# A Fourier mixing layer and two feed-forward layers on one core: the first element's DMA queue, keep-warm counts and weight-pair slots rearranged

## The reference

```python
def reference(x, filt_r, filt_i, w_in, w_out, alpha, w2_in, w2_out):
    # x: 2 x 3008 x 256, float32
    X = np.fft.rfft(x, axis=1)
    y = np.fft.irfft(X * (filt_r + 1j * filt_i)[None], n=3008, axis=1)
    t = y.reshape(6016, 256)
    h = t @ w_in                                  # 256 x 2048
    t = (np.maximum(h, 0) + alpha * np.minimum(h, 0)) @ w_out
    h = np.maximum(t @ w2_in, 0)
    return (h * h) @ w2_out
```

## Time and profile before

| | us |
|---|---|
| median of 3 runs (lowest to highest) | 1151.18 (1150.83 to 1153.68) |
| the profiled execution, its own time | 1149.17 |
| its span, first to last instruction | 1147.4 |
| TensorE busy | 1122.2 (98% of the span) |
| VectorE busy | 956.7 (83%) |
| ScalarE busy | 655.5 (57%) |
| GpSimd busy | 592.8 (52%) |

### The profile page before, as it was taken

How to read it: one execution, slowest core, us unless ns; L and a number is a source line. 1 busy time by engine, 2 the same in 40 slices (tenths; PEclk the granted TensorE clock), 3 DMA queues, 4 the chain that set the end, 5 groups by cost and what they waited for, 6 DMA issues and landing times.

```text
span 1147.4 us, 17088 instructions
## 1 busy us (share of the span) xinstructions
PE 1122.2 (98%) x6867; PEld 980.2 (85%) x6867; DVE 956.7 (83%) x1110; ACT 655.5 (57%) x769; POOL 592.8 (52%) x434
## 2 busy tenths in 40 slices
PE   7979999999999999999999999999999999999997
PEld 3456888888899999999999899999999999999996
DVE  0659788897989888888988988888888898888987
ACT  4737556565655556555556556555565555555553
POOL 0405544656555565565565654555455455555443
PEclk9999999999999999999999999999999999999999
DMA  9874352453204313312216801101100110110100
GB/s 260 267 232 117 83 137 70 117 127 96 58 29 133 83 51 83 83 51 83 83 51 225 313 7 37 37 1 36 37 16 22 36 36 1 37 37 1 37 19 18
DMA packets 63296, 93.16 MB, mean 81 GB/s; under 512 B 5232, under 2 KB 50288, under 8 KB 63216
## 3 DMA queue, kind: packets, MB, share of 16 engines
q1 hardware_dynamic: 63216, 92.06, 27.5%
HBM read 55.60 MB, written 36.44 MB: 80 GB/s over the span
## 4 chain that ended last, share of the span: by engine, by line
PE 90%; DVE 5%; issue 3%; POOL 1%; DMA 1%; ACT 1%; DVEq 0%; SPq 0%; PEldq 0%; POOLq 0%
PE bank L892 14%; PE bank L897 14%; PE bank L893 14%; PE bank L920 13%; PE bank L918 13%; PE bank L930 13%; PE bank L870 3%; DVE g_lo L739 1%; PE bank L830 1%; PE bank L832 1%; PE bank L844 1%; PE bank L838 1%; DVE g_raw L758 1%; DVE w_lo L685 1%; PE bank L812 1%
## 5 line engine op out<-in xcount | busy, mean ns | idle before, releaser
L485 POOL TENSOR_TENSOR g_raw<-g_raw 128x250 f32<-128x250 f32 (+1 forms) x191 | 279.6, 1464 | 468.4 <-DVE g_raw L768 468.4
L739 DVE TENSOR_TENSOR g_lo<-g_raw,g_hi 128x1750 fp32r<-128x1750 f32 (+1 forms) x192 | 417.6, 2175 | 44.3 <-ACT g_hi L497 43.1
L592 ACT ACTIVATE g_raw<-bank 128x500 f32<-128x500 f32 (+1 forms) x384 | 226.7, 591 | 339.9 <-PE bank L897 299.1
L497 ACT ACTIVATE g_hi<-g_raw 128x1750 fp32r<-128x1750 f32 (+1 forms) x192 | 320.3, 1668 | 42.3 <-POOL g_raw L488 39.8
L920 PE MATMUL bank<-g_hi,w_lo 128*128 128x250 f32 (+1 forms) x1344 | 321.7, 279 | 0.0
L918 PE MATMUL bank<-g_hi,w_hi 128*128 128x250 f32 (+1 forms) x1344 | 321.1, 279 | 0.0
L892 PE MATMUL bank<-in_hi,w_hi 128*128 128x500 f32 (+1 forms) x768 | 307.4, 400 | 6.2 <-DVE g_raw L758 6.2
L893 PE MATMUL bank<-in_hi,w_lo 128*128 128x500 f32 (+1 forms) x768 | 298.7, 389 | 0.0
L920 PEld LDWEIGHTS bank<-g_hi,w_lo 128*128 128x128 f32 x1344 | 254.1, 189 | 7.5
L918 PEld LDWEIGHTS bank<-g_hi,w_hi 128*128 128x128 f32 x1344 | 253.8, 189 | 7.4
L488 POOL TENSOR_TENSOR g_raw<-g_raw 128x250 f32<-128x250 f32 (+1 forms) x191 | 250.5, 1312 | 15.0
(11 more groups left out here) (60 smaller groups left out, 524.8 us busy)
## 6 DMA issues: line engine op xcount, KB each, us to landing
filt_b<-filt SPq DMA_DIRECT2D x36, 256.0 KB, 4.8
vc<-v_rows SPq DMA_DIRECT2D x24, 288.0 KB, 6.0
v_rows<-v_out_b SPq DMA_DIRECT2D x24, 256.0 KB, 2.5
w_rows<-s_hi SPq DMA_DIRECT2D x8, 704.0 KB, 3.1
w_rows<-s_lo SPq DMA_DIRECT2D x8, 704.0 KB, 3.1
w_hi<-w_rows SPq DMA_DIRECT2D x8, 704.0 KB, 5.4
w_lo<-w_rows SPq DMA_DIRECT2D x8, 704.0 KB, 6.8
w_raw<-w SPq DMA_DIRECT2D x8, 512.0 KB, 9.0
```

The costliest lines, as they stand in the source:

```text
L485: pool.tensor_tensor(g_raw[:, r, T2, 0:h], g_raw[:, r, B22, 0:h], g_raw[:, r, T1N, 0:h], ALU.add).then_inc(t2_ready, 1)
L497: return act.activation(dst, src, ACT.Copy)
L592: act.activation(g_raw[:, r, 2 * j:2 * j + 2, 0:h], h_ps[j][:, 0:2 * h].rearrange("p (j d) -> p j d", j=2), ACT.Relu, scale=-1.0 if n < SL ...
L739: dve.tensor_tensor(g_lo[:, q, B11:T4 + 1, 0:h], g_raw[:, q, B11:T4 + 1, 0:h], g_hi[:, q, :, 0:h], ALU.subtract).then_inc(g_lo_ready, 1)
```

## The change

It does these things. (1) SP's order in the first element's part: the filter part 0 goes ahead of the sign table and the rest of the constants, `const_y` and `alpha` go behind filter part 4, the store of units 8 and 9 goes behind chunks 0 and 1 and filter part 1, filter part 5 goes behind chunk 3, filter part 6 behind chunk 4. VectorE and TensorE wait on three semaphores (`const_raw_loaded`, `const_loaded`, `late_loaded`) in place of one. (2) Weight pair 0 is loaded after the tenth store of `v`, pair 1 after the last, and the first four column loads of `f1` come after one and two further pairs. (3) Two weight pairs (`EARLY_W` = 2) are made ahead of the loop; slot n makes pair n + 2 whole, its sums right behind L768. (4) `A_SLOT` uses slots 0 to 4 and 6 to 8 in place of 1 to 4 and 6 to 9. (5) `WARM_T` is 3 wide and 12 narrow matmuls in place of 8 wide, `WARM_V` 24 in place of 32.

```diff
--- before
+++ after
@@ -67,14 +67,15 @@
...
-A_SLOT = [s for s in (1, 2, 3, 4, 6, 7, 8, 9) for _ in range(2)]
+A_SLOT = [s for s in (0, 1, 2, 3, 4, 6, 7, 8) for _ in range(2)]
 B_SLOT = [12 + 2 * u for u in range(B_UNITS)]
 VC_P, Y_P, IN_P = 3, 5, 6
-EARLY_W, FIRST_W = 3, 2
+EARLY_W = 2
 W2_SLOT = [37, 43, 50, 58, 66, 74, 82, 90]
...
-WARM_X, WARM_T, WARM_V = 7, 8, 32
+WARM_X, WARM_T, WARM_V = 7, 3, 24
+WARM_NARROW = 12
 PRIME = 4
@@ -213,7 +214,8 @@
...
-        const_a_loaded, const_loaded = sem("const_a_loaded"), sem("const_loaded")
+        const_a_loaded, const_raw_loaded = sem("const_a_loaded"), sem("const_raw_loaded")
+        const_loaded, late_loaded = sem("const_loaded"), sem("late_loaded")
         const_ready = sem("const_ready")
@@ -301,48 +303,53 @@
...
+            def store_group(u):
+                store_t(f0, u, u % f0.outs)
+
             sp.dma_start(const_full[0:ROWS, 0:ROWS], consts_full[0:ROWS, 0:ROWS]).then_inc(const_a_loaded, 16)
-            ahead = 5
-            for u in range(0, ahead * f0.group, f0.group):
+            for u in range(0, A_HALF, f0.group):
                 load_x(f0, u)
-            sp.dma_start(const_raw[:, :], consts).then_inc(const_loaded, 16)
+            sp.dma_start(const_raw[:, :], consts).then_inc(const_raw_loaded, 16)
+            load_x(f0, A_HALF)
             for u in range(0, A_HALF, f0.group):
-                store_t(f0, u, u)
-                if u + ahead * f0.group < A_UNITS:
-                    load_x(f0, u + ahead * f0.group)
+                store_group(u)
+                if A_HALF + f0.group + u < A_UNITS:
+                    load_x(f0, A_HALF + f0.group + u)
+            load_filter(f0, 0, 0)
+            sp.dma_start(sign_sb[:, :], sign).then_inc(const_loaded, 16)
             sp.dma_start(const_full[:, ROWS:FULL_COLS], consts_full[:, ROWS:FULL_COLS]).then_inc(const_loaded, 16)
-            sp.dma_start(const_y_sb[:, :], const_y).then_inc(const_loaded, 16)
-            sp.dma_start(sign_sb[:, :], sign).then_inc(const_loaded, 16)
-            sp.dma_start(alpha_sb[:, :], alpha).then_inc(const_loaded, 16)
-            load_filter(f0, 0, 0)
-            store_t(f0, A_HALF, 0)
...
             load_chunk(1)
-            store_t(f0, A_HALF + 2, 2)
             load_filter(f0, 1, 1)
+            store_group(A_HALF)
+            store_group(A_HALF + 2)
             load_chunk(2)
-            store_t(f0, A_HALF + 4, 4)
             load_filter(f0, 2, 2)
-            store_t(f0, A_HALF + 6, 6)
-            for n in range(3, B_HALF):
-                load_filter(f0, n, n)
+            store_group(A_HALF + 4)
+            store_group(A_HALF + 6)
+            load_filter(f0, 3, 3)
+            load_filter(f0, 4, 4)
+            sp.dma_start(const_y_sb[:, :], const_y).then_inc(late_loaded, 16)
+            sp.dma_start(alpha_sb[:, :], alpha).then_inc(late_loaded, 16)
             for s in f0.a_stored:
...
             load_chunk(3)
+            load_filter(f0, 5, 5)
+            load_chunk(4)
             load_filter(f0, 6, 6)
-            load_chunk(4)
             load_filter(f0, 7, 7)
...
                     load_filter(f0, n + f0.filters, n)
-            for p in range(FIRST_W):
-                load_w1(p)
+                if n == B_UNITS - 3:
+                    load_w1(0)
+            load_w1(1)
@@ -357,10 +364,11 @@
...
             load_vc(0)
-            for p in range(FIRST_W, FP):
+            for p in range(EARLY_W, FP):
                 load_w1(p)
-                if p < FIRST_W + f1.xs:
-                    load_x(f1, p - FIRST_W)
+                for u in (2 * (p - EARLY_W), 2 * (p - EARLY_W) + 1):
+                    if u < f1.xs:
+                        load_x(f1, u)
@@ -547,7 +555,7 @@
...
-            for p in range(FIRST_W):
+            for p in range(EARLY_W):
                 w_high(p)
@@ -566,8 +574,6 @@
...
             in_high(0)
-            for p in range(FIRST_W, EARLY_W):
-                w_high(p)
             for n in range(2 * SLOTS_1):
@@ -629,9 +635,8 @@
...
             dve.tensor_copy(zeros_r[:, :], zeros[:, :]).then_inc(zeros_ready, 1)
-            dve.wait_ge(const_loaded, 5 * 16)
+            dve.wait_ge(const_raw_loaded, 16)
             dve.tensor_copy(const[:, :], const_raw[:, :]).then_inc(const_ready, 1)
-            dve.tensor_scalar(rest_sb[:, :], alpha_sb[:, :], -1.0, 1.0, ALU.mult, ALU.add).then_inc(rest_ready, 1)
@@ -685,15 +690,17 @@
...
+            dve.wait_ge(const_loaded, 2 * 16)
             for n in range(B_UNITS):
...
-            w_sums(0)
-            for p in range(FIRST_W):
-                if p + 1 < FIRST_W:
-                    w_sums(p + 1)
+            dve.wait_ge(late_loaded, 2 * 16)
+            dve.tensor_scalar(rest_sb[:, :], alpha_sb[:, :], -1.0, 1.0, ALU.mult, ALU.add).then_inc(rest_ready, 1)
+            for p in range(EARLY_W):
+                w_sums(p)
+            for p in range(EARLY_W):
                 w_low(p)
@@ -740,10 +747,6 @@
...
             in_low(0)
-            for p in range(FIRST_W, EARLY_W):
-                w_sums(p)
-                w_low(p)
-            w_sums(EARLY_W)
             for n in range(2 * SLOTS_1):
@@ -776,6 +779,8 @@
...
+                if n + EARLY_W < FP:
+                    w_sums(n + EARLY_W)
                 if p == LAG - 1 and g > 0:
@@ -788,8 +793,6 @@
...
                     w_low(n + EARLY_W)
-                if n + EARLY_W + 1 < FP:
-                    w_sums(n + EARLY_W + 1)
                 for q in range(FP):
@@ -802,9 +805,9 @@
...
-            def keep_warm(count, ps):
+            def keep_warm(count, ps, cols=COLS):
                 for _ in range(count):
-                    pe.matmul(ps[:, :], zeros_r[:, 0:P], zeros_r[:, :], start=True, stop=True)
+                    pe.matmul(ps[:, 0:cols], zeros_r[:, 0:P], zeros_r[:, 0:cols], start=True, stop=True)
@@ -851,12 +854,15 @@
...
             keep_warm(WARM_T, f0.v_ps[0])
+            keep_warm(WARM_NARROW, f0.v_ps[0], PAIR_TOK)
             pe.wait_ge(const_ready, 1)
...
                     spectrum_0(n + f0.deep)
+                if n == 0:
+                    pe.wait_ge(const_loaded, 2 * 16)
                 inverse_0(n)
@@ -935,6 +941,7 @@
...
             pe.wait_ge(f0.v_ready, done(B_UNITS - 1))
+            pe.wait_ge(late_loaded, 2 * 16)
             y_group(0)
```

## The result

Timed beside each other in 17 runs each, the changed kernel takes 1155.40 us (median; 1152.74 to 1159.95) and the kernel before 1151.34 (1150.22 to 1154.32). The ratio is 1.0028, with a 95% interval of 1.0017 to 1.0039: slower, by 2 to 4.5 us. That is outside the predicted range and on the other side of its centre. The changed kernel's profiled execution took 1158.19 us (span 1156.4), the one of before 1149.17 (1147.4), so the two traces differ by 9.0 us where the medians differ by 4.1. The traces show where time went; how far they overstate it is taken up at the end of the experiments.

A forecast was written before the change was run, and what follows sets the result against it. Transfers and the first transform bound up to 72 us, VectorE from 72 to 111 us, TensorE behind that. Terms -0.6 - 1.3 + 0.3 + 0.4 = -1.2 us moved the 1151.18 us median to 1150.0, range 1146.2 to 1153.4.

The forecast's parts named there:

- signs of being wrong: Slots under 7.1 us, `y_group(0)` over 4, chunk 2 used before 30 or after 32.5, TensorE newly idle behind slot 7.
- Part 1, the head: SP's queue: chunk 2 lands 0.3 us sooner and chunk 3 0.3 us more; -0.6 us, bounds -2.2 and +0.7.
- ahead of chunk 2 stands the same set of transfers as before: Head: transfers ahead of chunk 2 unchanged, less two constants of 43 KB, in a full queue; 0.3 us taken for chunk 2.
- The bound of +0.7: Head: if the queue runs dry while SP waits for stores ahead of chunk 0, chunk 2 is up to 1 us later.
- Part 2, vc: Load of vc: one weight pair less ahead of it in the queue; -1.3 us, bounds -1.85 and 0.
- rival C: Queue before vc: `v` stores are delayed as much as vc gains, so vc lands as before; 1151.3 us, chance 0.13.
- Part 3, the clock: First group: fewer keep-warm matmuls and earlier vc leave TensorE idle 0.7 us longer; +0.3 us, bounds 0 and +3.5.
- rival A: `y_group(0)` and `up(0)` at 1.2 GHz: +3.3 in place of +0.3; 1153.0 us, 1154.3 with late chunk 2; chance 0.17.
- the clock held for 5 us after the last keep-warm matmul: First group: the old trace's full clock after keep-warm ended, given as the argument against rival A.
- Part 4, the slots: Slots 0 to 6: `up(7)` +2.1 from one weight pair a slot, `A_SLOT` -1.7; together +0.4 us, bounds -5.6 and +1.8.
- it starts at 126.5 and ends 1.72 later: Slot 6: TensorE's transform waits for the input's low part, done at 126.4, then `up(7)` starts at 128.2, +2.1 us.
- rival B: VectorE's slots shorten to 7.05 us as GpSimd disturbs less; 1147.2 us, 1144.0 with no GpSimd cost; chance 0.20.

The follow-up runs named there:

- changed again: The changed kernel run once more with nothing edited: 1156.21 us, ratio 1.0024 to the kernel before.
- experiment 9: Changed kernel with 42 keep-warm matmuls ahead of the first group and no unit in slot 6, SP's head order as changed: 1149.19 us, ratio 0.9978.
- Experiment 1: Changed kernel with SP's order in the head put back as before: 1154.68 us, ratio 1.0016 to the kernel before.
- experiment 8: Changed kernel with 42 keep-warm matmuls, no unit in slot 6, and the store of units 8 and 9 ahead of SP's wait: 1149.86 us, ratio 0.9983.
- experiment 3: Changed kernel with 42 keep-warm matmuls ahead of the first group in place of 24: 1152.32 us, ratio 0.9987 to the kernel before.
- experiment 5: Kernel before with only the change's new slot table `A_SLOT`: 1150.99 us, ratio 0.9982 to the kernel before.
- experiment 7: Changed kernel with weight pair 1 loaded behind vc and 42 keep-warm matmuls: 1154.31 us, ratio 1.0012 to the kernel before.
- 2: Changed kernel with the second element's first-step units in slots 0 to 4 and 7 to 9, none in slot 6: 1153.20 us, ratio 1.0001.

## Why the prediction was wrong

The forecast was 1150.0 us, range 1146.2 to 1153.4, and 1155.4 was measured. Its way of summing, shifts up to the moment at which TensorE becomes the bound, held: behind slot 9 all traces agree within 0.7 us. Of its signs of being wrong two came, chunk 2 used at 35.65 us and a `y_group(0)` of 5.30. Of its terms two were mis-sized, one had the wrong sign, and the fourth was right in its mechanism and missed what follows from it.

**Part 1, the head: -0.6 predicted, +2.1 measured.** The failing step is "ahead of chunk 2 stands the same set of transfers as before". It counted bytes in a full queue and not the time in which SP issues. In the old order the store of units 8 and 9 was issued ahead of SP's wait, where SP would stand idle anyway, and one store group stood between the chunks. In the new one both groups do, and four stores in a row took 3.75, 4.26 and 3.21 us to issue (changed, changed again, experiment 9), and everything behind them went out later, chunk 2 first and then the stores that SP's second wait stands for. The 0.3 us that the prediction gave chunk 3 for one filter part less ahead of it had the wrong sign with it: chunk 3 was issued 14.29 us behind the first transform in place of 12.43. The bound of +0.7, for a queue that runs dry while SP waits, is not what the traces show: from chunk 0's issue to chunk 2's the DMA share was 0.92 in the changed kernel and 0.94 before, and from there to chunk 2's use 1.06 and 1.00. Experiment 1 undid the late issue together with the rest of the order, and experiment 8, by the one store, has chunk 2 and chunk 3 as early as the old order has them. A second mechanism is seen in the chains: in six of the eight traces with parts 5 to 7 issued behind SP's second wait, one of these late parts stands on the path (8.45, 7.85, 8.27, 7.92, 7.96 and 5.89 us from issue to landing), and in none of the six traces with parts 3 to 5 ahead of that wait. That is a correlation, and it fits the 1.0 us that lie behind chunk 3's issue; but no run changed the order of the filter parts alone, so the share of the filter parts is argued and not shown. Nor is the head's loss shown in the timed runs: wherever two kernels differ in the head's order alone, the intervals of their ratios overlap.

**Part 2, vc: -1.3 predicted, about -0.4 measured** (9.2 us over the ten traces with the new load order, 9.66 over the four with the old one, which differ by as much among themselves). The chains show its two parts. vc, from its second issue to its landing, took 4.8 to 6.4 us with one pair directly ahead (5.6 on average) and 6.3 to 7.2 with two (6.5): 0.9 us won, where the prediction chose 1.3 between 1.1 and the distance of two landings, 1.85. And the step that put the delay of the last `v` stores at nothing in the sum failed: the last store landed after 2.47 to 2.51 us in the four traces of the old order and after 2.88 to 3.13 in nine of the new, which takes 0.5 us back. The prediction had this as its bound of 0 and as rival C, at full size; it came in a little over half.

**Part 3, the clock: +0.3 predicted, +2.1 measured.** Here rival A is what happened: `y_group(0)` wholly at 1.2 GHz, 5.30 us against the 5.75 it gave, and 1.4 us more in slot 0 (experiment 3), which the four segments book under the slots. The prediction saw that the idle stretch grows and counted 0.7 us for it; it became 4.92 in place of 2.80. Eight matmuls less are 1.8 of these 2.1 us (24 of them took 6.03 us and 42 took 10.11), and vc, which was to come 1.3 us earlier, came 0.3 us later behind the last `v` copy in this trace. The failing step is the term itself, which let the half clock begin about where it had begun before, near the end of `y_group(0)`. The argument against rival A, that "the clock held for 5 us after the last keep-warm matmul", came from one trace. In experiment 5, with the old 32 keep-warm matmuls, the same stretch is at a mean of 0.74:

```profile
73.75:77.42 3.67, 3.67 (x25) 3.67 (x26) 1.50 (x2) 0.59 (x1) 0.00 (x0) 0.74 1.04 326
```

So the margin was thin before, and eight fewer removed it. Over the fourteen traces `y_group(0)` took 2.8 us behind idle stretches of up to 0.97 us, 3.05 behind 1.41, 3.20 and 3.68 behind 2.80 and 2.84, and 4.93 to 5.30 behind 3.66 to 4.98. The rule of the Trainium skill that stood beside this term ("TensorE: Matmul & The Clock Gate", section "HAM oscillation — how this bites in real kernels") says that waits for data bring the half clock back for the next burst. The first groups agree with it. Rival A deserved more than 0.17, the more so as the mend costs next to nothing, since the keep-warm matmuls fill an idle stretch: with 42 of them TensorE still waited 0.4 to 1.4 us for vc in five of seven traces, in experiment 3 they ended as it landed, and in experiment 7 they ran past its landing by 0.3 to 0.5 us. VectorE's first activation, which was to come 3 us earlier relative to vc, came 86.14 - 77.31 = 8.8 us behind vc's landing in place of 81.78 - 72.01 = 9.8, and 5.5 us behind it in experiment 3: the slow clock took most of that gain.

**Part 4, the slots: +0.4 predicted, +1.6 measured.** The timetable of VectorE held. The wait in slot 6 ends 133.38 - 84.09 = 49.3 us after `in_low(0)` by the trace and 49.8 by the prediction. Two of its steps erred against each other: a slot is 7.37 us and not 7.59, and slot 0 is 8.45 us and not 7.95. What failed is the step "it starts at 126.5 and ends 1.72 later", which took the old duration at full clock. The 1.76 us of idle were followed by 3.3 us at 0.54, which made the transform 0.85 us longer, and the matmuls of `up(7)` behind it about as much. That is the 1.7 us that `A_SLOT` had won. Experiment 5 confirms the win by itself (1.9), experiments 3 and 9 put the loss in slot 6 at 2.3 us with a warm first group, and the 1.4 us of slow clock in slot 0 are in this segment too: -1.9 + 2.3 + 1.4 = 1.8, against 1.6 measured. That the four matmuls would run slow was not certain: in experiment 7 they took 1.96 us behind the same wait, and why the clock held there is open.

**GpSimd.** Neither the 7.59 nor rival B came about. In the old order the two instructions that ran beside GpSimd's were `w_low` (2.16 us, 1.62 alone) and the first sum behind it, which took 0.82 us where it takes 0.29 alone:

```profile
93.41 0.82 DVE L669 SCALAR_TENSOR_TENSOR w_raw<-w_raw 128x128 f32<-128x128 f32 x1
```

In the new order both are free (1.61 and 0.29 us), and two other sums, which now run beside GpSimd's L493 and L496, take 0.72 and 0.71. So 0.54 + 0.53 us became 0.43 + 0.42, and the slot is 0.22 us shorter, not 0.54 or 1.09. The prediction used the rule of the Trainium skill, "Advanced Engine Details and Errata", section "Mode Summary", on instructions at double rate, as if no others paid anything; the rows show over 0.4 us on each of these sums, so the measurement decides again.

**The range.** Its upper end took rival A without a late chunk. All four terms erred the same way, and they are not independent: both the first group and slot 6 lose through the same thing, a wait that is followed by slow matmuls. The chances of 0.17 for rival A and 0.06 for a time over 1154.6 us treated late chunk, clock and slots as separate accidents.

## What to carry to other kernels

An idle stretch of TensorE is priced at its length plus the half-clock matmuls that may stand behind it; where a change shortens the filler or adds a wait, look at how near the old trace already was to that fall, in more than one run. What a DMA-issuing engine issues ahead of its own wait, where it would stand idle, costs it no time, and the same issues behind the wait delay everything that comes after them; so what is due late is not always best issued late. And a unit of work that waits on the lagging engine belongs in a slot in which that engine has caught up: keeping one pair of units out of slot 6 was worth 2.3 to 3.3 us by the traces (experiments 9 against 3, and 2 against the changed kernel).
